# An attention and two-layer expert kernel: first weights of the second group's slots named by its first token, slots three steps earlier

## The chip, the cores and the metric

One core of a Trainium2 chip. The metric is the time of one execution in microseconds, lower is better; three runs of the kernel before are given, with their median.

## The reference

Three stages follow each other.

```python
# attention: q, k, v of 2 batches, 8 heads, 576 rows, 64 columns; top_k = 32
scores = scale * np.matmul(q, k.transpose(0, 1, 3, 2))
kth = np.partition(scores, -top_k, axis=-1)[..., -top_k:-top_k + 1]
scores = np.where(scores >= kth, scores, -1000000000.0)
attn = softmax(scores); x = attn @ v            # as x [1152, 512]
# first experts: one of 8 for each token
logits = x @ w_gate + modality_bias[modality_id]
e_idx = np.argmax(logits, axis=1)
out[mask] = gate_w[mask, None] * (np.maximum(x[mask] @ w1[e], 0.0) @ w2[e])
# second experts: all 4 for each token, weighted by domain_probs / sum
out += p[:, e:e + 1] * (np.maximum(x @ w1[e], 0.0) @ w2[e])
```

The hidden width is 1024, so one expert has w1 of 512x1024 and w2 of 1024x512, 2 MB each.

## The kernel before, in words

The 1152 tokens are nine tiles of 128. Attention runs over 72 "heads" g (nine query tiles of eight heads) in a loop of 78 steps p on each engine. In step p PE computes the scores of head p, multiplies head p-6 by the values and transposes head p-5. DVE finds the 32nd largest score of two heads at a time (find_thresholds, fourteen MAX8 and MATCH_REPLACE8 a pair), GpSimd masks (mask), ACT copies and takes exponents. Each engine has a generator beside(), advanced once a step (on DVE once behind each of the fourteen instructions, a clock of steps/7), which puts other work between the heads at written-out steps: A_START, TOKENS_AT and the like. Where no such work is due, PE multiplies v_one by itself (keep_dense, the filler).

The experts' tokens are sorted in two groups. Group A is tiles 0 to 2, and its first five slots (128 rows of one expert each, plain f32 matmuls) run inside the heads loop. A slot s takes seven steps from A_START + 7 s: a_x (transposes of gathered rows, a step ahead), up parts in three steps (3, 3 and 2 of eight), two a_turn (transposes), down parts in two steps (4 and 4); ACT copies between them (a_copy_xT, a_relu_half, a_copy_hT, a_copy_y). PE's clock inside the loop is held at step 75 and ACT's at 76, so that what is due later waits until the loop is over.

Group B is tiles 3 to 8. Its routing can only be finished with the last tile: pick finds each token's expert, ranks and more_ranks count tokens by matmuls with triangular matrices, place computes rows and slots of tokens, sum_tokens gives the list of tokens of each slot (tokens_made). Experts with tokens are served in the order of their numbers (kth_expert). Then GpSimd gathers the rows of the first two slots (gather_slot), PE transposes them (turn_slot), and each slot is computed with operands split in a rounded high part and a low part: ACT rounds (split_high, w1_high), DVE subtracts (split_low, w1_split), three matmuls for each product. Weights come through one raw buffer for w1 and one for w2, which group A's slots use too. SP issues the loads in program order: first_up for the first w1, held at its third quarter until tokens_made; w2 once the first rows have landed. Behind the slots come the four experts of the last stage for all tokens.

The seam from the last logits to slot 0 reads on PE:

```python
            last_logits()
            clock.now = AV_END - 1
            advance(work_beside)          # the fifth slot's last two up parts
            more_ranks(GB, GB.tiles - 1, 3)
            clock.now = AV_END + 2
            advance(work_beside)          # its two a_turn and four down parts
            sum_tokens(GB)
            clock.now = 1000
            for _ in work_beside:         # the other four down parts
                pass
```

## Time and profile before

| what | value |
|---|---|
| median of 3 runs | 943.93 us (943.23 to 944.47) |
| profiled execution, whole | 945.33 us |
| its span | 943.6 us |
| mean granted clock of PE | 0.962 |
| PE busy | 903.5 us, 96% of the span |
| DVE busy | 560.5 us, 59% |
| ACT busy | 340.5 us, 36% |
| GpSimd (POOL) busy | 280.8 us, 30% |

The rows are of the profiled execution, which took 945.33 us in all with a span of 943.6 from its first to its last instruction. Busy shares are means over stages: the heads loop ends near 416 us, group B's slots begin near 435 us and the last stage near 540 us. A granted clock of 1.00 is 2.4 GHz, one of 0.50 is 1.2 GHz. In the rows, an engine's time is followed by a line of the kernel, the operation, and output and inputs by name; a bracket gives the engine's idle time ahead of it and what ended that.

### The profile page before, as it was taken

The numbers are of one execution on the slowest core, as the hardware profiler recorded it, in microseconds if no ns is written. First come the engines' busy times: TensorE is split into PE (matmuls) and PEld (weight loads), VectorE is DVE, ScalarE is ACT, GpSimd is POOL, SyncE is SP. The second block draws the span as 40 slices with busy tenths as digits, with TensorE's granted clock in tenths as the row PEclk, the third lists the DMA queues.
The fourth block names the chain that finished last, engine by engine and source line by source line (L and its number), as shares of the span: only waits on it lengthen the run. The fifth ranks groups of instructions, "written<-read, shape, count | busy, mean of one in ns | idle before, by whom it ended". The sixth has DMA issues, their size and how long they took to land.

```text
span 943.6 us, 13457 instructions
## 1 busy us (share of the span) xinstructions
PE 903.5 (96%) x4823; PEld 758.8 (80%) x4823; DVE 560.5 (59%) x1097; ACT 340.5 (36%) x726; POOL 280.8 (30%) x227
## 2 busy tenths in 40 slices
PE   4999999998999999996999799999999999999998
PEld 4888888886676676764778689989998999889897
DVE  4999999999999998935544523324223421332121
ACT  3545555554454663524543412303112220222010
POOL 7576657655667666303111210000000000000000
PEclk8589999998899999997999899999999999999999
DMA  9130000005034353338916250022002200000001
GB/s 220 39 124 23 1 24 12 12 13 201 15 109 136 124 176 113 102 117 310 344 34 223 74 198 1 1 89 90 1 1 90 84 5 0 0 0 0 33 11 56
DMA packets 49396, 75.63 MB, mean 80 GB/s; under 512 B 24624, under 2 KB 24624, under 8 KB 49328
## 3 DMA queue, kind: packets, MB, share of 16 engines
q1 hardware_dynamic: 42160, 61.09, 19.1%
q0 software_dynamic: 4160, 13.63, 4.4%
q8 instruction: 36, 0.59, 0.3%
q10 hardware_dynamic: 3008, 0.05, 0.2%
q14 instruction: 32, 0.26, 0.1%
HBM read 63.49 MB, written 11.27 MB: 79 GB/s over the span
## 4 chain that ended last, share of the span: by engine, by line
PE 76%; DVE 17%; DMA 2%; issue 2%; POOL 1%; ACT 1%; SPq 0%; ACTq 0%; DVEq 0%; POOLq 0%
PE bank L1339 19%; PE bank L1341 18%; PE bank L1340 18%; DVE work L1038 7%; PE bank L1395 6%; DVE top L1043 5%; PE bank L1467 4%; PE bank L1334 3%; PE bank L1483 3%; PE bank L1366 2%; DVE top L1029 2%; PE bank L1364 1%; PE bank L1496 1%; DMA b_xs_raw<-x_dram,b_tok_i 1%; DMA w_raw<-in_moe_w_dram 1%
## 5 line engine op out<-in xcount | busy, mean ns | idle before, releaser
L620 POOL TENSOR_SCALAR att<-sc,top 128x576 f32<-128x576 f32 x70 | 120.6, 1723 | 122.5 <-DVE top L1043 119.8
L1043 DVE MAX8 top<-work 128x8 f32<-128x576 f32 x216 | 152.1, 743 | 0.1
L1339 PE MATMUL bank<-xT,w1h 128*128 128x384 f32 x384 | 129.6, 338 | 5.3 <-DVE w1l L1218 5.3
L1276 DVE SCALAR_TENSOR_TENSOR hT<-bank,hT 128x384 fp32r<-128x384 f32 x96 | 53.0, 557 | 131.0 <-ACT hT L940 129.0
L1341 PE MATMUL bank<-xT,w1h 128*128 128x384 f32 x384 | 129.1, 336 | 0.0
L1340 PE MATMUL bank<-xT,w1l 128*128 128x384 f32 x384 | 129.1, 336 | 0.0
L940 ACT ACTIVATE hT<-bank 128x384 fp32r<-128x384 f32 x96 | 46.9, 491 | 200.9 <-PE bank L1341 199.3
L1339 PE MATMUL bank<-w2h,hT 128*128 128x512 f32 x288 | 112.2, 390 | 1.2 <-DVE hT L1276 1.2
L1395 PE MATMUL bank<-v_one,attT 128*128 128x65 f32 (+3 forms) x800 | 111.8, 280 | 0.8 <-ACT av L752 0.6
L1341 PE MATMUL bank<-w2l,hT 128*128 128x512 f32 x288 | 112.2, 390 | 0.0
L1340 PE MATMUL bank<-w2h,hT 128*128 128x512 f32 x288 | 112.2, 389 | 0.0
L1395 PEld LDWEIGHTS bank<-v_one,attT 128*128 128x128 f32 (+3 forms) x800 | 97.7, 188 | 17.0 <-issue 9.3
L1038 DVE MATCH_REPLACE8 work<-top,work 128x576 f32<-128x576 f32 x144 | 106.3, 744 | 0.0
L623 POOL TENSOR_TENSOR att<-att,ex 128x576 f32<-128x576 f32 x70 | 98.8, 1412 | 7.2 <-ACT ex L738 1.6
L1288 DVE SCALAR_TENSOR_TENSOR x_tok<-bank,pr_e,x_tok 128x512 f32<-128x512 f32 x27 | 20.3, 751 | 115.0 <-PE bank L1341 115.0
L744 ACT ACTIVATE attT<-bank 128x512 f32<-128x512 f32 x72 | 43.0, 597 | 105.1 <-PE bank L1366 105.1
L1339 PEld LDWEIGHTS bank<-xT,w1h 128*128 128x128 f32 x384 | 72.8, 189 | 6.0 <-DVE w1l L1218 5.7
L1340 PEld LDWEIGHTS bank<-xT,w1l 128*128 128x128 f32 x384 | 72.8, 189 | 0.3
L1341 PEld LDWEIGHTS bank<-xT,w1h 128*128 128x128 f32 x384 | 72.6, 189 | 0.0
L729 ACT ACTIVATE sc<-bank 128x576 f32<-128x576 f32 x72 | 46.6, 647 | 68.4 <-PE bank L1341 68.4
L1339 PEld LDWEIGHTS bank<-w2h,hT 128*128 128x128 f32 x288 | 54.1, 188 | 12.5 <-DVE hT L1276 1.5
L1341 PEld LDWEIGHTS bank<-w2l,hT 128*128 128x128 f32 x288 | 54.0, 188 | 11.3
(253 smaller groups left out, 1520.4 us busy)
## 6 DMA issues: line engine op xcount, KB each, us to landing
w_raw<-in_moe_w_dram SPq DMA_DIRECT2D x96, 512.0 KB, 6.3
q_raw<-in_q_dram SPq DMA_DIRECT2D x18, 128.0 KB, 2.6
v_one<-in_v_dram POOLq DMA_DIRECT2D x18, 128.0 KB, 5.6
out_dram<-x_tok SPq DMA_DIRECT2D x9, 256.0 KB, 2.0
k_raw<-in_k_dram SPq DMA_DIRECT2D x8, 256.0 KB, 5.2
y_dram<-zero POOLq DMA_DIRECT2D x2, 1024.0 KB, 6.7
y_dram<-b_ys POOLq DMA_DIRECT2D x7, 256.0 KB, 3.4
x_dram<-x_cur SPq DMA_DIRECT2D x6, 256.0 KB, 2.1
```

The lines of the kernel that those rows point to most:

```text
L620: nc.gpsimd.tensor_scalar(att[:, g % ATR, :], sc[:, g % RING, :], top8[:, g % RING, 3, 7:8], None, ALU.is_ge).then_inc(keep_made, 1)
L623: nc.gpsimd.tensor_tensor(att[:, g % ATR, :], att[:, g % ATR, :], ex[:, g % EXR, :], ALU.mult).then_inc(att_made, 1)
L729: nc.scalar.activation(sc[:, g % RING, :].rearrange("p (a b) -> p a b", a=2), bank[:, SB:SB + 2, 0:HS], ACT.Copy, scale=float(D) ** -0.5). ...
L744: nc.scalar.activation(attT[:, g % 2, 0:KC - 1, :].rearrange("p c q -> p (c q)"), bank[:, TBK, :], ACT.Copy)
L940: nc.scalar.activation(hTh(b)[:, f, :], bank[:, HB + f % 4, 0:BW], ACT.Relu).then_inc(h_high, 1)
L1038: nc.vector.match_replace(out=work[:, j, :], in_to_replace=top8[:, g % RING, i, :], in_values=sc[:, g % RING, :] if i == 0 else work[:, j, ...
L1043: nxt = nc.vector.max(out=top8[:, g % RING, i + 1, :], in_=work[:, j, :])
L1276: nc.vector.scalar_tensor_tensor(out=hTl(b)[:, f, :], in0=bank[:, HB + f % 4, 0:BW], scalar=0.0, in1=f32(hTh(b)[:, f, :]), op0=ALU.max, op ...
L1339: nc.tensor.matmul(dst, high_lhs, high_rhs, start=start, stop=False)
L1340: nc.tensor.matmul(dst, low_lhs, high_rhs, start=False, stop=False)
L1341: return nc.tensor.matmul(dst, high_lhs, low_rhs, start=False, stop=stop)
L1395: last = nc.tensor.matmul(bank[r0:r1, AVB, 0:W], attT[0:kk, g % 2, c, r0:r1], v_one[b][0:kk, h, c, :], start=(c == 0), stop=(c == KC - 1))
```

## The change

Five things are changed together.

1. Group B's experts are numbered from the expert of its first token on (turn_experts): DVE takes that token's expert out of the first four tiles' pick, PE spreads it over all partitions by a matmul with a one-row matrix (spread_first, in step 72), and DVE makes from it first_i and the turned numbers that one-hots are compared with. place turns kth_expert back, now behind the slot tables.
2. SP's first_up waits for first_made instead of the second group's experts_made, and has no pause at the third quarter. The store of the last x tile moves behind it. ke is read behind the waits ahead of the first w2 load.
3. A_START goes from 46 to 43, TOKENS_AT from 42 to 40, place on DVE starts 0.6 step earlier and its second part is asked for at TOKENS_AT - 1.8; x transposes and logits of tiles 3 to 6 come two steps later.
4. On PE more_ranks of the last tile follows last_logits directly. With the slots three steps earlier, the fifth slot's up parts and a_turn are now inside the heads loop, and its down parts are what stands around sum_tokens.
5. GpSimd makes the low part of the first two w1 quarters; DVE makes that of the other two. ACT rounds all four at once, ahead of the first rows' copy and behind the beside work, and takes the second group's Exp behind that work too. The rare slots beyond the fifth move out of the generators.

```diff
@@ -208,9 +213,9 @@
         RING, EXR, ATR = 8, 4, 3
-        EXP_LAG, TR_LAG, AV_LAG, X_LAG, L_LAG = 2, 5, 6, 17, 18
+        EXP_LAG, TR_LAG, AV_LAG = 2, 5, 6
         STEPS = HEADS + AV_LAG
-        RANKS_AT, TOKENS_AT, A_START, A_STEP, SPREAD = 37, 42, 46, 7, 5
+        RANKS_AT, TOKENS_AT, A_START, A_STEP, SPREAD = 37, 40, 43, 7, 5
         HB, HTB, YB, XB = 0, 2, 4, 7
...
@@ -218,11 +223,15 @@
 
-        def x_at(p, lag):
-
-            t = (p - lag) // H
-            return t if p >= lag and (p - lag) % H == 0 and t < T - 1 else None
-
+        def x_at(p):
+
+            return next((t for t in range(T - 1) if p == t * H + (19 if TB <= t < T - 2 else 17)), None)
+
+        def logits_at(p):
+            return x_at(p - 1)
+
+        FIRST_AT = HEADS
+        AV_END = HEADS + AV_LAG - 1
         turn_use = {}
...
@@ -236,14 +245,14 @@
                 next_use("ql", low)
-            if x_at(p, X_LAG) is not None:
-                next_use("x", x_at(p, X_LAG))
-            if x_at(p, L_LAG) is not None:
-                next_use("lg", x_at(p, L_LAG))
+            if x_at(p) is not None:
+                next_use("x", x_at(p))
+            if logits_at(p) is not None:
+                next_use("lg", logits_at(p))
+            if p == FIRST_AT:
+                next_use("first", 0)
         next_use("x", T - 1)
         next_use("lg", T - 1)
-
-        AV_END = HEADS + AV_LAG - 1
 
...
@@ -466,13 +477,11 @@
 
-            def load(e, kth, raw, src, split, loaded, pause=False):
+            def load(e, kth, raw, src, split, loaded):
                 sp.wait_ge(split, kth * DC + BASE)
...
                 for c in range(DC):
-                    if pause and c == 2:
-                        sp.wait_ge(GB.tokens_made, 2)
                     sp.dma_start(raw[:, c * n:(c + 1) * n, :], rows[:, c * n:(c + 1) * n, :]).then_inc(loaded[c], 16)
...
@@ -483,8 +492,8 @@
             def first_up():
-                sp.wait_ge(GB.experts_made, 2)
-                load(expert_of(0), 0, w1_raw, w1, w1_split, w1_loaded, True)
+                sp.wait_ge(first_made, 1)
+                load(sp.value_load(first_i[0:1, 0:1], min_val=0, max_val=E - 1), 0, w1_raw, w1, w1_split, w1_loaded)
 
...
@@ -501,6 +510,7 @@
                 with sp.If(guarded(sp, GA, SPREAD)):
+                    keep_x(T - 1)
                     a_store(SPREAD - 1)
...
@@ -518,6 +528,7 @@
                     first_up()
+                    keep_x(T - 1)
                     a_store(SPREAD - 1)
...
@@ -536,21 +547,20 @@
                 clock.now = p
-                if x_at(p, X_LAG) is not None:
-                    keep_x(x_at(p, X_LAG))
+                if x_at(p) is not None:
+                    keep_x(x_at(p))
                 low = q_at(p)[1]
...
                 advance(work_beside)
-            keep_x(T - 1)
             clock.now = 1000
...
 
+            sp.wait_ge(a_d, GA.slots)
+            sp.wait_ge(slot_loaded[0], 16)
             ke = sp.value_load(GB.table_i[0:1, 1, E:E + 1], min_val=1, max_val=E)
-            sp.wait_ge(slot_loaded[0], 16)
-            sp.wait_ge(a_d, GA.slots)
             load(expert_of(0), 0, w2_raw, w2, w2_split, w2_loaded)
...
@@ -637,11 +650,6 @@
                 yield from clock.until(1000)
-                with pool.If(guarded(pool, GA, SPREAD)):
-                    for s in range(SPREAD, GA.slots):
-                        with pool.If(guarded(pool, GA, s)):
-                            a_gather(s)
-                            pool.sem_inc(passed, 1)
                 pool.wait_ge(a_stored, 16 * GA.slots)
...
@@ -657,6 +665,14 @@
                 advance(work_beside)
+            with pool.If(guarded(pool, GA, SPREAD)):
+                for s in range(SPREAD, GA.slots):
+                    with pool.If(guarded(pool, GA, s)):
+                        a_gather(s)
+                        pool.sem_inc(passed, 1)
+            for c in range(2):
+                pool.wait_ge(w1_high, c + 1)
+                nc.gpsimd.tensor_tensor(w1l[:, c, :], w1_raw[:, c, :], f32(w1h[:, c, :]), ALU.subtract).then_inc(w1_split, 1)
             pool.wait_ge(x_kept, 16 * T)
...
@@ -815,24 +831,22 @@
                 a_copy_y(SPREAD - 1)
-                yield from clock.until(1000)
-                with act.If(guarded(act, GA, SPREAD)):
-                    for s in range(SPREAD, GA.slots):
-                        with act.If(guarded(act, GA, s)):
-                            a_copy_xT(s)
-                            a_relu_half(s, 0)
-                            a_relu_half(s, 1)
-                            a_copy_hT(s, 0)
-                            a_copy_hT(s, 1)
-                            a_copy_y(s)
-                            act.sem_inc(passed, 1)
-                        with act.Else():
-                            act.drain().then_inc(a_xT_copied, 1)
-                            act.drain().then_inc(a_relu, 2)
-                            act.drain().then_inc(a_hT_copied, 2)
-                            act.drain().then_inc(a_ys, 1)
-                with act.Else():
-                    act.drain().then_inc(a_ys, GA.slots - SPREAD)
+
+            def a_rare_slots():
+                for s in range(SPREAD, GA.slots):
+                    with act.If(guarded(act, GA, s)):
+                        a_copy_xT(s)
+                        a_relu_half(s, 0)
+                        a_relu_half(s, 1)
+                        a_copy_hT(s, 0)
+                        a_copy_hT(s, 1)
+                        a_copy_y(s)
+                        act.sem_inc(passed, 1)
+                    with act.Else():
+                        act.drain().then_inc(a_xT_copied, 1)
+                        act.drain().then_inc(a_relu, 2)
+                        act.drain().then_inc(a_hT_copied, 2)
+                        act.drain().then_inc(a_ys, 1)
 
...
@@ -870,19 +884,24 @@
                     act.wait_ge(zero_set, 1)
-            read_rest_of_x()
-            act.wait_ge(GB.lsub_made, 3)
-            nc.scalar.activation(GB.lg_b[:, :, :], GB.lg_a[:, :, :], ACT.Exp).then_inc(GB.lexp_made, 1)
-            clock.now = 1000
-            for _ in work_beside:
-                pass
-
             def split_high(kth, raw, high, loaded, done, parts=range(DC)):
...
                     nc.scalar.activation(high[:, c * n:(c + 1) * n, :], raw[:, c * n:(c + 1) * n, :], ACT.Copy).then_inc(done, 1)
+
+            read_rest_of_x()
+            clock.now = 1000
+            for _ in work_beside:
+                pass
+            act.wait_ge(GB.lsub_made, 3)
+            nc.scalar.activation(GB.lg_b[:, :, :], GB.lg_a[:, :, :], ACT.Exp).then_inc(GB.lexp_made, 1)
+            with act.If(guarded(act, GA, SPREAD)):
+                a_rare_slots()
+            with act.Else():
+                act.drain().then_inc(a_ys, GA.slots - SPREAD)
+            split_high(0, w1_raw, w1h, w1_loaded, w1_high)
 
...
@@ -919,12 +938,10 @@
 
-            split_high(0, w1_raw, w1h, w1_loaded, w1_high, (0, 1))
             act.wait_ge(GB.table_made, 2)
...
             slot_xT(0)
-            split_high(0, w1_raw, w1h, w1_loaded, w1_high, (2, 3))
             split_high(0, w2_raw, w2h, w2_loaded, w2_high)
...
@@ -1099,8 +1116,23 @@
                     dve.wait_ge(g.rank_made, 1)
-                nc.vector.tensor_tensor(g.onehot[:, a:b, :], over_e(g.lidx[:, a:b], n), over_t(ecol_less[:, :], n), ALU.is_equal).then_inc(g.hot_made, 1)
+                if g is GB and part == 1:
+                    yield from turn_experts(step)
+                names = turned_less if g is GB else ecol_less
+                nc.vector.tensor_tensor(g.onehot[:, a:b, :], over_e(g.lidx[:, a:b], n), over_t(names[:, :], n), ALU.is_equal).then_inc(g.hot_made, 1)
                 yield
+
+            def turn_experts(step):
+
+                nc.vector.tensor_copy(first_less[:, :], GB.lidx[:, 0:1]).then_inc(first_seen, 1)
+                yield from clock.until(HEADS - 1.6)
+                dve.wait_ge(turn_made, turn_use["first", 0])
+                nc.vector.tensor_copy(first_less[:, :], bank[:, TXB, 0:1]).then_inc(turn_read, 1)
+                dve.wait_ge(turn_read, turn_use["first", 0])
+                nc.vector.tensor_scalar(first_i[:, :], first_less[:, :], float(E), None, ALU.add).then_inc(first_made, 1)
+                step(nc.vector.tensor_scalar(turned_less[:, :], ecol[:, :], first_less[:, :], None, ALU.add))
+                step(nc.vector.tensor_scalar(turned_by[:, :], turned_less[:, :], 0.0, -float(E), ALU.is_ge, ALU.mult))
+                step(nc.vector.tensor_tensor(turned_less[:, :], turned_less[:, :], turned_by[:, :], ALU.add))
 
...
@@ -1111,7 +1143,7 @@
                 step(nc.vector.tensor_reduce(out=g.lidx[:, t:t + 1], in_=g.lg_a2[:, t, :], axis=AX.X, op=ALU.min))
-                nc.vector.tensor_scalar(g.onehot[:, t, :], ecol_less[:, :], g.lidx[:, t:t + 1], None, ALU.is_equal).then_inc(g.hot_made, 1)
+                nc.vector.tensor_scalar(g.onehot[:, t, :], turned_less[:, :], g.lidx[:, t:t + 1], None, ALU.is_equal).then_inc(g.hot_made, 1)
                 nc.vector.tensor_scalar(g.lg_a[:, t, :], lp, g.lmax[:, t:t + 1], None, ALU.subtract).then_inc(g.lsub_made, 1)
...
@@ -1133,7 +1165,8 @@
                 step(nc.vector.tensor_reduce(out=g.kth_expert[:, :], in_=g.cmp_kth[:, :, :], axis=AX.X, op=ALU.add))
-                nc.vector.tensor_copy(g.kth_expert_i[:, :], g.kth_expert[:, :]).then_inc(g.experts_made, 1)
+                if g is GA:
+                    nc.vector.tensor_copy(g.kth_expert_i[:, :], g.kth_expert[:, :]).then_inc(g.experts_made, 1)
                 yield
...
@@ -1161,6 +1194,10 @@
                 nc.vector.tensor_copy(g.by_slot_i[:, 1, :], g.by_slot[:, 1, :]).then_inc(g.table_made, 1)
+                if g is GB:
+                    step(nc.vector.tensor_scalar(g.kth_expert[:, :], g.kth_expert[:, :], first_less[:, :], None, ALU.add))
+                    step(nc.vector.tensor_scalar(turned_by[:, :], g.kth_expert[:, :], 0.0, float(E), ALU.is_lt, ALU.mult))
+                    nc.vector.tensor_tensor(g.kth_expert_i[:, :], g.kth_expert[:, :], turned_by[:, :], ALU.add).then_inc(g.experts_made, 1)
                 yield from tokens_asked
...
@@ -1175,8 +1212,8 @@
                 yield from pick(GA, 0, TB, 1)
-                yield from clock.until(RANKS_AT - 0.4)
-                yield from place(GA, 1, clock.until(TOKENS_AT - 2.2))
+                yield from clock.until(RANKS_AT - 1)
+                yield from place(GA, 1, clock.until(TOKENS_AT - 1.8))
                 yield from clock.until(HEADS - 4)
...
@@ -1261,9 +1298,9 @@
             ke = dve.value_load(GB.table_i[0:1, 1, E:E + 1], min_val=1, max_val=E)
-            split_low(0, w1_raw, w1h, w1l, w1_high, w1_split, (0, 1))
+            dve.wait_ge(w1_split, 2 + BASE)
+            split_low(0, w1_raw, w1h, w1l, w1_high, w1_split, (2, 3))
             slot_xT_low(0)
-            split_low(0, w1_raw, w1h, w1l, w1_high, w1_split, (2, 3))
             split_low(0, w2_raw, w2h, w2l, w2_high, w2_split)
...
@@ -1406,6 +1443,13 @@
                 last.then_inc(turn_made, 1)
+
+            def spread_first():
+
+                pe.wait_ge(first_seen, 1)
+                pe.wait_ge(zero_set, 3)
+                take_turn("first", 0)
+                nc.tensor.matmul(bank[:, TXB, 0:1], first_row[:, :], first_less[:, :], start=True, stop=True).then_inc(turn_made, 1)
 
...
@@ -1628,17 +1672,17 @@
                     transpose_att(p - TR_LAG)
-                if x_at(p, L_LAG) is not None:
-                    x_logits(x_at(p, L_LAG))
+                if logits_at(p) is not None:
+                    x_logits(logits_at(p))
                 advance(work_beside)
+                if p == FIRST_AT:
+                    spread_first()
                 if p == HEADS + 2:
...
             last_logits()
+            more_ranks(GB, GB.tiles - 1, 3)
             clock.now = AV_END - 1
-            advance(work_beside)
-            more_ranks(GB, GB.tiles - 1, 3)
-            clock.now = AV_END + 2
             advance(work_beside)
...
```

## Rows read from the trace of the kernel before

**Rows 1.** Busy time by stretch: PE, PEld, DVE, ACT, POOL, PEclk, DMA share, GB/s

```profile
245.00:264.50 19.50, 19.50 (x84) 13.12 (x82) 19.50 (x42) 9.29 (x25) 13.51 (x10) 0.82 0.09 29
...
245.30:416.30 171.00, 169.88 (x920) 120.11 (x918) 151.68 (x325) 87.77 (x223) 96.24 (x64) 0.98 0.36 120
...
429.20:434.70 5.50, 0.00 (x0) 0.00 (x0) 2.36 (x2) 2.60 (x3) 0.09 (x1) 0.85 0.83 229
434.70:443.40 8.70, 7.15 (x19) 5.49 (x20) 6.02 (x6) 5.66 (x6) 4.53 (x4) 0.51 0.84 293
...
448.20:453.70 5.50, 5.50 (x24) 4.57 (x25) 4.81 (x6) 4.62 (x6) 0.23 (x1) 1.00 1.03 406
```

**Rows 2.** Chain of waits over the seam: start us, us, what

```profile
416.31 3.40 PE bank L1467 x4
...
420.09 0.21 DVE b_cmp_cnt L1124
...
423.78 0.96 DVE b_row_hot L1153
...
427.00 7.62 DMA b_xs_raw<-x_dram,b_tok_i
...
444.50 1.06 ACT w2h L885
```

**Rows 3.** Timelines of DVE, ACT and PE in the seam: start us, us, engine

```profile
417.01 0.23 DVE L1114 TENSOR_SCALAR b_onehot<-ecol_less,b_lidx 128x8 f32<-128x8 f32 x1
...
431.71 2.36 DVE L1218 TENSOR_TENSOR w1l<-w_raw,w1h 128x1024 fp32r<-128x1024 f32 x2 [4.93 <-ACT w1h L885]
...
417.40 0.24 ACT L875 ACTIVATE b_lg_b<-b_lg_a 128x48 f32<-128x48 f32 x1 [1.64 <-DVE b_lg_a L1115]
...
429.20 0.60 ACT L792 ACTIVATE ys<-bank 128x512 f32<-128x512 f32 x1 [7.52 <-PE bank L1483]
430.62 2.00 ACT L885 ACTIVATE w1h<-w_raw 128x1024 fp32r<-128x1024 f32 x2 [0.82 <-issue]
...
425.49 3.68 PE L1483 MATMUL bank<-w_raw,hsT 128*128 128x512 f32 x8
```

**Rows 4.** Groups of instructions on GpSimd: busy us, mean ns | idle us

```profile
L623 POOL TENSOR_TENSOR att<-att,ex 128x576 f32<-128x576 f32 x70 | 98.8, 1412 | 7.2 <-ACT ex L738 1.6
...
L577 POOL TENSOR_TENSOR q_raw<-q_raw,q_high 128x512 f32<-128x512 f32 x9 | 11.5, 1279 | 4.3 <-ACT q_high L706 4.3
```

**Rows 5.** Timelines of PE and GpSimd around steps 41 to 45

```profile
218.99 1.11 PE L1334 MATMUL bank<-ident,x_cur 128*128 128x128 f32 x4 [4.59 <-DVE x_cur L1067]
...
229.90 0.40 PE L1339 MATMUL bank<-kTh,qTh 64*128 64x288 f32 x1
...
233.19 1.04 PE L1496 MATMUL bank<-v_one 128*128 128x260 f32 x4
...
244.25 0.30 PE L1364 MATMUL bank<-ident,att 128*64 128x128 f32 x1 [1.87 <-POOL att L623]
...
222.64 1.41 POOL L623 TENSOR_TENSOR att<-att,ex 128x576 f32<-128x576 f32 x1
```

**Rows 6.** Gathers to landing: all of xs_raw, b_xs_raw at 427.0, at 473.7

```profile
DMA to landing us min/median/max: 3.4/6.3/7.1
...
b_xs_raw<-x_dram,b_tok_i POOLq DMA_INDIRECT x1, 7.6
...
b_xs_raw<-x_dram,b_tok_i POOLq DMA_INDIRECT x1, 3.4
```

**Rows 7.** Timelines of PE and DVE near the loop's end

```profile
392.03 0.60 PE L1334 MATMUL bank<-ident,x_cur 128*128 128x128 f32 x4
...
400.08 0.96 PE L1407 MATMUL bank<-wg,gxT 128*128 128x8 f32 x8
...
406.41 0.30 PE L1364 MATMUL bank<-ident,att 128*64 128x128 f32 x1
...
387.47 1.41 DVE L1029 MAX8 top<-sc 128x8 f32<-128x576 f32 x2
```

26 lines of the change are left out of this document (18 added, 8 removed).

## The prediction

> **What bounds the kernel now.** I read the busy time by stretch first [rows 1]. Between 245.3 and 416.3 us, the last 32 steps of the heads loop with the first group's slots woven in, PE is busy 169.88 of 171.00 us: it is the bound, so PE work moved inside this stretch keeps its price. Behind it comes the seam to the second group's slots: 429.2 to 434.7 has no PE work at all, and 434.7 to 443.4 has a granted clock of 0.51, the 1.2 GHz level of the two (1.2 and 2.4).
>
> Then the chain of waits over the seam [rows 2]. The last logits end at 416.3; slot matmuls of 3.40 us stand ahead of the ranks; DVE places the tokens from 420.09 on, with the rows' one-hot done at 424.74; GpSimd issues the first row gather at 427.00, and it is the transfer, 7.62 us, that PE waits for. The timelines of the engines [rows 3] show what stands beside: the last matmul of the first group ends at 429.17 (425.49 + 3.68), ACT copies ys until 429.80, and only at 430.62 rounds the first w1 quarter; DVE subtracts from 431.71. Today none of this is last, as w1 is ready before the gathered rows are.
>
> **Part 1: two w1 quarters go to GpSimd, ahead of the gather.** This is the part that decides. In GpSimd's program the new loop waits for the first and second w1_high and subtracts each quarter; only behind it stand the waits for the tokens and gather_slot(0). On ACT, w1_high still comes behind all of the beside work, whose last piece, a_copy_y of the fifth slot, waits for a_d, the end of that slot's eight down parts. PE issues the second four of them behind sum_tokens, as before. So w1, fetched early, isn't rounded early. The chain to the gather becomes: down parts, ys, the second group's Exp (now behind ys), w1h, two subtractions on GpSimd, gather.
>
> Its length [rows 3]: ys ends 0.63 after the down parts; 0.82 of issue as today; Exp 0.24; w1h until who waits for it can start 1.09 (430.62 to 431.71). The subtraction of 128x1024 on GpSimd is not in the trace. The nearest rows are the same operation on 128x512 (1279 ns) and 128x576 (1412 ns) [rows 4]: 2.08 ns an element, so 1024 take 1.28 + 512 x 0.00208 = 2.35 us; by doubling it would be 2.56. The low end is DVE's 1.2 for this shape (two in 2.36 [rows 3]), which GpSimd reaches in no row. I take 2.35, twice, 4.7; the second w1h is hidden under the first subtraction. With 0.3 to issue: 0.63 + 0.82 + 0.24 + 1.09 + 4.7 + 0.3 = 7.8 us from the end of the down parts to the gather. There is a rule on this choice of engine: the Trainium skill, "GPSIMD Engine Reference", Engine selection, gives two-input elementwise work to VectorE, GpSimd being about twice as slow. By it a subtraction is 2 x 1.2 = 2.4 us and the chain 0.1 longer; it speaks against this part, and the two rows bear it out.
>
> **Part 2: slots three steps earlier, ranks ahead of the last portion.** How does the end of the down parts move? I keep a ledger of PE from the start of step 43, now 229.90 [rows 5].
> - The first slot's transposes now stand in step 42 and wait for its rows. GpSimd can issue that gather behind mask 37, whose product ends at 224.05 (222.64 + 1.41), so at 224.4. The 4 MB of weights, issued some 5 us earlier than now, are still in flight. This gather took 6.3 as a median, bounds 3.4 and 7.1 [rows 6]. Rows at 230.7, transposes 0.6: step 43 starts at 231.3, +1.4.
> - Dense filler of steps 43 and 44 goes, 1.0 each: -2.0. The idle 1.87 at 244.25 is filled: -1.9. The 0.6 of transposes is now ahead of step 43: -0.6.
> - x transposes and logits of tile 3, two steps later than now, fall into 43 and 44: 0.5 + 0.8 [rows 7] = +1.3.
> - Two up parts and eight transposes now stand ahead of the last logits. By the rate of the down parts (3.68 for eight) four such matmuls are 1.8 at full clock (3.4 today in the seam, where the clock drops), the transposes 0.9: +2.7.
> - spread_first, one small matmul: 0.3; in step 76 nothing but the last heads covers ACT's copy of attT: some 0.4: +0.7.
>
> Sum +1.6: the last logits end near 418.0. The low clock behind 244.25 (0.82 over 19.5 us [rows 1], so 7.0 us at half speed, 3.5 lost) I leave in, since PE idles ahead of step 43 instead. Behind the logits PE waits 0.93 for DVE's last one-hot (416.31 to 417.24 today), the ranks and the hand-over take 0.6: DVE starts to place at 419.5, against 420.09. Then 4.7 to sum_tokens as now, 0.7 for it, 3.7 for the last down parts: they end at 428.6 against 429.2. What three steps of lead gain is nearly all paid back, as PE is the bound on both sides: -0.6.
>
> DVE's new work: turn_experts has six instructions like the 0.23 of 417.01, 1.2 us with their waits, and the second of them waits for PE's step 72. PE reaches its end some 6 us after DVE's place, since it has steps 71 and 72 with three up parts each in between. DVE idles so long; behind it are eleven passes of 0.70 (the rest of the pair and the first product), 7.7 + 1.2 = 8.9 us. PE has from step 73 to head 70's transposes 392.03 to 406.41 now, 14.4 [rows 7], of which 7.0 is slot work (3.7 + 2.8 + 0.5) that shrinks to 2.4: 9.8. So the wait is covered, by 0.9. The three instructions put ahead of tokens_made (0.5 us) leave it near 427, 9 us ahead of the gather; nobody waits.
>
> **Part 3: the gather and slot 0.** The gather starts at 428.6 + 7.8 = 436.4, 9.4 later than now. But the w1 load is over by then, and w2 is held until these rows land: the gather runs with no weights beside it. Today's took 7.6 us with w1 quarters in flight; a later one with the queues empty took 3.4 [rows 6]. A second gather follows 1.3 us behind, so I take 3.6, bounds 3.4 and 7.6: rows at 440.0 against 434.6, +5.4. What follows is as now, the low clock after an idle stretch too. w2's first issue has one register load more ahead of it (0.3) and less traffic beside it; the chain goes through w2's rounding (444.50) with the up parts ending beside it, so half a microsecond either way: nothing.
>
> **Part 4: the new numbering.** The slots of an expert are filled by its own tokens, so their number and that of weight sets stay. Changes of expert fall ahead of other slots, perhaps twice in succession. Ahead of slot 1 that is so today, a slot after the first load, and PE is busy 5.50 of 5.50 us up to it [rows 1]. Nothing.
>
> **Sum.** -0.6 for the down parts, +10.0 for the gather (427.0 was 2.2 ahead of their end and is now 7.8 behind), -4.0 for its transfer: +5.4 us. The rows are of an execution with a span of 943.6 that took 945.33 in all; the median of three is 943.93, and I add to that: **949.3 us**.
>
> **Rivals.**
> - *PE's slack is worth all it shows* (the other side). Idle 4.59 and 1.87, four fillers of 1.04 and 3.5 of low clock between 212 and 264 [rows 1, 5], 14 us, would leave the path and the down parts end that much earlier: 943.9 + 6.0 - 14 = 936. It decides from about 8 us. Against it: PE's idle at 218.99 is a wait for DVE's x_cur, and heads 36 to 39 are held by DVE whatever PE does. 0.06.
> - *Half of it is*: the first slot's gather lands soon enough, step 43 starts as now and PE doesn't cool, 1.4 + 3.5 less: 944.4, no change to be measured. 0.12.
> - *The gather stays slow*: four more gathers are issued within 6 us behind it. At 7.6 us: 953.3. 0.14. The Trainium skill, "DMA: Bandwidth & Descriptors", Latency and other measured facts, has HBM latency at 2 us under load and 0.2 without: by that the gather would gain 1.8 and the time be 951.5. The row of 3.4 says more.
> - *DVE's new wait comes on the path*: its cover is 0.9 of a sum of a dozen terms. Without it most of the 6 us shows in the last logits, about 954. 0.10.
> - The forecast has 0.58. That the change doesn't do what it says is part of it: nobody waited for w1, so its early fetch alone is worth nothing.
>
> **How the numbers follow.** A measurement of this kernel tells 0.2%, 1.9 us, from no change: 942.0 to 945.8. From the cases: faster 0.06, within 0.12, slower 0.82. The range goes from 945, into the half case, to 955, past the slow gather and DVE's wait; some 0.12 is left below and 0.05 above. The forecast's own range, from the subtraction's 2.56 and a step or two of PE, is 947 to 952.
>
> **What would show it.** GpSimd: two subtractions of about 2.35 us ending just ahead of the first b_xs_raw gather, near 436, which lands in under 4 us. ACT: w1h behind ys, though w1 landed before 415. PE: idle some 11 us ahead of slot 0. DVE: a wait of several us in the last pair of heads. I am wrong if the down parts end before 422, if w1h comes ahead of them, or if the gather takes 7 us.

## The result, and the profile after

The changed kernel takes 956.09 us as a median (953.17 to 961.23, four executions) against 943.73 us for the kernel before in the same measurement: ratio 1.0136, 95% interval 1.0091 to 1.0181. It is slower, by 12.4 us, where the forecast had 5.4 and the range ended at 955. The profiled execution has a span of 951.4 us against 943.6, so 7.8 of the 12.4 are in this trace; the rest lies between executions.

Busy time of the changed kernel by stretch (PE, PEld, DVE, ACT, POOL, granted clock, DMA share, GB/s); the fourth row answers to the idle stretch in [rows 1], the fifth to the one behind it:

```profile
229.90:245.30 15.40, 15.40 (x90) 10.98 (x89) 15.40 (x35) 7.47 (x18) 12.97 (x9) 0.82 0.06 18
245.30:416.10 170.80, 169.33 (x957) 120.47 (x955) 148.67 (x323) 90.14 (x227) 93.52 (x62) 1.00 0.38 132
416.10:428.20 12.10, 11.12 (x27) 5.42 (x26) 7.00 (x34) 0.00 (x0) 0.00 (x0) 0.72 0.04 15
428.20:440.10 11.90, 0.12 (x1) 0.00 (x0) 2.93 (x5) 4.62 (x6) 8.42 (x5) 0.72 0.18 51
440.10:453.70 13.60, 8.81 (x28) 6.63 (x28) 4.80 (x5) 5.30 (x7) 2.99 (x4) 0.75 0.94 335
```

PE has nothing to do for 11.9 us where it had nothing for 5.5. The timelines of ACT, POOL, PE and SP in the seam, to be laid beside [rows 3]:

```profile
417.98 6.24 PE L1527 MATMUL bank<-w_raw,hsT 128*128 128x512 f32 x8
...
428.36 0.60 ACT L808 ACTIVATE ys<-bank 128x512 f32<-128x512 f32 x1 [12.68 <-PEq L1591]
428.85 0.23 ACT L899 ACTIVATE b_lg_b<-b_lg_a 128x48 f32<-128x48 f32 x1
429.77 3.90 ACT L892 ACTIVATE w1h<-w_raw 128x1024 fp32r<-128x1024 f32 x4 [0.69 <-issue]
430.91 4.64 POOL L675 TENSOR_TENSOR w1l<-w_raw,w1h 128x1024 fp32r<-128x1024 f32 x2 [37.00 <-ACT w1h L892]
435.59 2.36 DVE L1255 TENSOR_TENSOR w1l<-w_raw,w1h 128x1024 fp32r<-128x1024 f32 x2 [5.83 <-POOL w1l L675]
435.71 2.02 POOL L680 DMA_INDIRECT b_xs_raw<-x_dram,b_tok_i  x1 [0.16 <-issue]
...
440.23 1.09 PE L1371 MATMUL bank<-ident,b_xs_raw 128*128 128x128 f32 x4 [11.91 <-DMA b_xs_raw<-x_dram,b_tok_i]
441.46 14.99 SPq L485 DMA_DIRECT2D w_raw<-in_moe_w_dram  x12
```

ACT waits 12.68 us for the last down part while w1, whose four loads were all issued by 404.4 and landed within 6.3 us, lies ready; the rounding follows, then the two subtractions (2.32 us each), and only then the gather. PE waits 11.91 us for it. The chain of waits shows the two transfers and what stands between them, beside [rows 2]:

```profile
435.71 4.38 DMA b_xs_raw<-x_dram,b_tok_i
...
440.17 0.27 SPq L563
...
443.18 8.98 DMA w_raw<-in_moe_w_dram
...
452.18 1.06 ACT w2h L892
453.24 0.49 ACT b_hs L927
```

The rows land 5.5 us later than before (440.09 against 434.62), but w2's last quarter is rounded 7.7 us later (452.18 against 444.50 [rows 2]), and the relus come behind it. Beside w2's fetch stand the first group's token gathers (x_tok). In the kernel before, the first of them came 1.39 us behind w2's first issue at 435.34; in the changed kernel, whose first issue is at 441.46, it comes 2.17 us ahead of it. The fetch and the first gather of the kernel before, then the gathers of the changed kernel:

```profile
437.05 7.43 DMA w_raw<-in_moe_w_dram
...
436.73 0.95 POOL L647 DMA_INDIRECT x_tok<-y_a,a_pos_i  x1 [7.44 <-DMA y_a<-ys]
```

```profile
439.29 0.95 POOL L655 DMA_INDIRECT x_tok<-y_a,a_pos_i  x1 [0.31 <-issue]
440.55 0.95 POOL L655 DMA_INDIRECT x_tok<-y_a,a_pos_i  x1 [0.30 <-issue]
441.80 0.95 POOL L655 DMA_INDIRECT x_tok<-y_a,a_pos_i  x1 [0.30 <-issue]
```

### The profile page after: what moved, and what is told of

Read it like the earlier page. It is cut to its first block, busy times and chain, and to the rows that moved or that the text cites. A ratio compares the mean times of both kernels' runs of the same rounds, so it can differ in the third digit from the quotient of the medians.

```text
span 951.4 us, 13448 instructions
## 1 busy us (share of the span) xinstructions
PE 903.7 (95%) x4813; PEld 758.7 (80%) x4813; DVE 557.8 (59%) x1103; ACT 340.6 (36%) x726; POOL 286.1 (30%) x231
## 4 chain that ended last, share of the span: by engine, by line
PE 75%; issue 10%; POOL 9%; DMA 3%; SPq 1%; DVE 1%; ACT 1%; PEld 1%; PEldq 0%; POOLq 0%; DVEq 0%; ACTq 0%
PE bank L1376 19%; PE bank L1377 18%; PE bank L1378 18%; PE bank L1432 6%; POOL att L633 6%; PE bank L1511 4%; PE bank L1371 4%; PE bank L1527 3%; POOL att L636 2%; PE bank L1403 2%; PE bank L1401 1%; DMA w_raw<-in_moe_w_dram 1%; DMA q_raw<-in_q_dram 1%; DMA xs_raw<-x_a,a_tok_i 1%; PE bank L1540 1%
```

## The experiments

All times are medians of all executions; each ratio is against the kernel before on the same chip, with a 95% interval. It can differ by up to 0.2% from the quotient of the two medians. "Profile" is one execution of each. The runs are on three chips, so a step between two kernels of different chips is better read from the ratios.

**The changed kernel again**, to have it on one chip with the next two and the first of those that hold w1 back:

> The changed kernel, unchanged. Its profile showed a span of 951.4 us, but its other executions took 955 to 961. If the spread lies in the seam (where the w2 load, the gathers and the next w1 load meet), this profile shows the last w2 quarter landing at another distance from its issue than 10.7 us, and the rest of the kernel, from slot 0's first down product on, at 494.8 us as before. If it lies in the last stage instead, that stretch differs. Median expected: 956, lowest to highest 6 us or more apart, while the kernel before stays within 1.5.

955.78 us, ratio 1.0103 (1.0077 to 1.0130), the kernel before 944.64. The profiled execution is a middle one, span 954.8: 3.4 us more than the profile shown above. 2.0 are there at 308.9 us already (the transposes of one of the first group's row blocks start at 308.88 instead of 306.92), 1.6 at slot 0's first down product (457.86 instead of 456.27), and 1.8 come behind that, where the granted clock from 455 to 500 us is 0.93 instead of 0.97. The seam isn't where the two differ, and the kernel before doesn't stay within 1.5 us as expected: its 23 executions are 7.3 us apart (941.8 to 949.1).

**GpSimd's subtractions behind the first two gathers:**

```
-for c in range(2): (wait for w1_high; w1l[:, c] = ...)   # GpSimd
 gather_slot(0)
 gather_slot(1)
+for c in range(2): (wait for w1_high; w1l[:, c] = ...)
```

> The changed kernel with GpSimd's two subtractions moved behind the first two gathers. Queue theory (the gather waits for work put ahead of it on GpSimd): gather at 425.8 instead of 435.7, rows at about 430; then slot 0 waits for the rest of the w1 split on DVE (end 438) and starts near 438.7 against 442.8; w2 issued 10 us earlier lands by 441 and no longer delays the down parts, which start near 449.5 against 456.6: 7 us off the changed kernel, about 949. Rival, that the loss lies in the heads loop (DVE's wait for step 72, slots moved): the time stays at 956 and only idle time shifts.

947.38 us, ratio 1.0031 (1.0008 to 1.0053): 8.4 us less than the changed kernel, 6.8 by the two ratios. The gather and the turn of its rows:

```profile
427.74 1.05 POOL L677 DMA_INDIRECT b_xs_raw<-x_dram,b_tok_i  x1 [32.02 <-DVE b_pos_i L1204]
...
431.30 0.63 PE L1371 MATMUL bank<-ident,b_xs_raw 128*128 128x128 f32 x4 [1.73 <-DMA b_xs_raw<-x_dram,b_tok_i]
```

Part 1 has its price shown: what stands ahead of the gather on GpSimd is most of the loss.

**ScalarE rounds the first w1 as soon as the last x is read**, subtractions left ahead of the gather:

```
 read_rest_of_x()
+split_high(0, w1_raw, w1h, w1_loaded, w1_high)
 (the rest of the first group)
```

> The changed kernel with ACT's rounding of the first w1 moved ahead of the last beside work (the copy of ys), all else the same. Queue theory: w1h at 415.8 to 419.7, subtractions on GpSimd end near 421.5, before the tokens are known at 425; the gather goes at 425.8, rows near 430, slot 0 at 432.8 against 442.8, down parts near 444 to 445 against 456.6: 12 us off, about 943 or somewhat below the kernel before (938 to 943). Heads-loop rival: no better than 950.

946.72 us, ratio 1.0021 (1.0003 to 1.0039), where 938 to 943 was expected. That is 9.1 us less than the changed kernel: rounding early takes off the same wait as moving the subtractions, so the two gains are one and don't add. The gather comes at 429.29, 3.5 us later than expected. 1.4 of that are there before the tokens are placed (the one-hot step starts at 418.25 here, at 416.82 in the changed kernel's profile). For the other 2 the timelines say why, first of this kernel:

```profile
417.93 4.66 POOL L675 TENSOR_TENSOR w1l<-w_raw,w1h 128x1024 fp32r<-128x1024 f32 x2 [22.94 <-ACT w1h L892]
...
418.25 2.06 DVE L1146 TENSOR_SCALAR b_onehot<-turned_less,b_lidx 128x8 f32<-128x8 f32 x1
...
421.98 0.78 DVE L1160 TENSOR_TENSOR b_cmp_pre<-below,b_counts 128x144 f32<-128x144 f32 x1
```

and the same two VectorE steps in the kernel with the gather first, where GpSimd is idle beside them:

```profile
419.00 0.23 DVE L1146 TENSOR_SCALAR b_onehot<-turned_less,b_lidx 128x8 f32<-128x8 f32 x1
...
420.90 0.31 DVE L1160 TENSOR_TENSOR b_cmp_pre<-below,b_counts 128x144 f32<-128x144 f32 x1
```

Beside GpSimd's subtractions a step of 0.23 us took 2.06, and it ends with the first of them; another took 0.78 instead of 0.31 and ends with the second. The six other VectorE steps beside them kept their lengths. All of them belong to the steps that make the token lists. VectorE's own two quarters then stood behind the Exp and were made at 434.75.

**All four low quarters on VectorE again:**

```
-for c in range(2): ...                          # GpSimd
-dve.wait_ge(w1_split, 2 + BASE)
-split_low(0, w1_raw, ..., (2, 3))
+split_low(0, w1_raw, ...)
```

> Undoes one part of the change alone: VectorE makes all four low quarters of the first w1, as before, and GpSimd makes none, so that the gather of slot 0 stands behind nothing but its tokens. Against the kernel with the two gathers ahead of GpSimd's subtractions (947.4 us): there VectorE waited for GpSimd until 436.9, made its two quarters by 439.2 and only then the low part of the rows (439.8). Theory (the seam is bound by what stands in one engine's line): the four quarters of 1.2 us each follow ScalarE's (431.0 to 434.9) and end at about 436.2, the low part of the rows at 437.0, first product 437.2 instead of 440.0, first down product about 2.5 us earlier; time about 945. Rival (GpSimd's help is worth its time, since VectorE has four subtractions of w2 to make as well): 947 to 948. A second rival (the second product waits for w2 and not for the rows): first product 3 us earlier but down product at the same place, time 947.

946.87 us, ratio 1.0032 (1.0018 to 1.0045). The first product starts at 437.98, 0.8 later than by the theory, the second at 447.11, 1.1 us before that of the kernel before; yet the median is 3 us above it. (The profiled execution took 945.65 us.) So the seam of one profile doesn't give the median any more, and the help of GpSimd is worth nothing measurable: 1.0032 against 1.0031.

**The first group's steps as before**, alone in the changed kernel:

```
-RANKS_AT, TOKENS_AT, A_START = 37, 40, 43    (x of tiles 3 to 6 at step 19)
+RANKS_AT, TOKENS_AT, A_START = 37, 42, 46    (x at step 17, and the other engines' steps)
```

> The changed kernel with the first group's steps as in the kernel before (ranks 37, tokens 42, first slot from 46, x of each tile at its step 17, and the steps of GpSimd, ScalarE and VectorE with them); all else as changed. Against the changed kernel on this chip (955.8). Theory A (the moved steps bring TensorE to the lower clock: 0.50 in 222 to 230 us and 0.70 to 0.82 in 230 to 245, where before it was 0.82 and 1.00): the loop over the heads ends 1 to 3 us earlier, time 953 to 955. Theory B (my ledger: the moved steps take 1.5 to 2 us of waits out of TensorE's line before the end of the down parts): time 957 to 958. Nothing in the seam itself changes by either.

960.25 us, ratio 1.0184 (1.0159 to 1.0209): 4 to 5 more than either measurement of the changed kernel. That is theory B's direction, 2 us above its range. In its profile eight transposes and sixteen down products are left behind the token sums, and ys comes at 432.97 instead of 428.36.

**These steps alone in the kernel before:**

> The kernel before, with only the first group's steps and the step of each x as in the changed kernel (tokens 40, first slot from 43, x of the tiles from the fourth to the seventh two steps later, ranks asked 0.6 of a step earlier); no new numbers, no early fetch of w1, no ranks ahead, GpSimd makes no low quarters. In the changed kernel these steps are worth 4.3 us (960.3 without them). Theory A (they take waits out of TensorE's line wherever they stand): down parts end 2 to 3 us earlier; the gather waits for the tokens at the same place as before, which come 1 to 2 us earlier too: time 941 to 943. Theory B (they pay only with the ranks ahead, since their other price is the lower clock of 222 to 245 us): 944 to 946.

949.90 us, ratio 1.0060 (1.0037 to 1.0082). Neither theory: it costs 5.8 us. Its timelines:

```profile
416.56 5.38 PE L1485 MATMUL bank<-w_raw,hsT 128*128 128x512 f32 x8
...
421.78 0.28 PE L1444 MATMUL bank<-b_onehot,before 128*128 128x8 f32 x2
...
425.86 0.60 ACT L794 ACTIVATE ys<-bank 128x512 f32<-128x512 f32 x1 [7.82 <-PE bank L1485]
...
429.23 1.05 POOL L666 DMA_INDIRECT b_xs_raw<-x_dram,b_tok_i  x1 [33.98 <-DVE b_pos_i L1169]
```

The down parts end 3.3 us earlier, as the theory has it, but eight of their products now stand ahead of the last ranks, where four up products stood [rows 2], so the ranks come 2.2 us later, and with them tokens and gather (429.23 against 427.00). Slot 0's first down product is 3.6 us later (451.74 against 448.18), 1.9 of it in w2's fetch, which took 9.28 us here instead of 7.43. The moved steps pay only with the ranks ahead. What the ranks ahead do by themselves isn't shown: no run has them alone.

**The next w1 held back until the first w2 is rounded; the three x_tok gathers behind slot 1; both together:**

```
+sp.wait_ge(w2_high, DC)                      # SyncE, ahead of the other experts' loads
 gather_slot(1)
-(gathers of x_tok)
+(slot(0), slot(1)), then (gathers of x_tok)  # GpSimd
```

> The changed kernel with SP holding the second expert's w1 load until the first w2 is rounded. Load theory (w2's 10.7 us to landing come from the next w1 load beside it): last w2 quarter lands 7 to 9 us after the first issue, slot 0's down parts start 2 to 3 us earlier, median 953. Rival, that the three x_tok gathers and the third row gather beside it make w2 late: 10 to 11 us as before, median unchanged at 956.

> The changed kernel with the three gathers of the first group's rows (x_tok) put behind GpSimd's work of slot 1, so that they no longer run beside the load of the first w2. Theory (the fetch of w2 took 10.7 us from first issue to last quarter because these gathers share the DMA engines with it, 200 to 250 GB/s where 400 were reached later): w2 lands within about 8.5 us of its first issue, the second product begins 1.5 to 2 us earlier, time about 954. Rival (the fetch is slow for itself, or the low clock of TensorE holds the product as long): w2's time stays 10 us or the down product stays where it was, time 956.

> The changed kernel with both loads kept from the fetch of the first w2: the gathers of the first group's rows behind slot 1, and the second expert's weights behind the rounding of w2. Each alone left the fetch at 9.0 and 10.4 us from first issue to last landing (10.7 in the changed kernel). If the two share it: about 7.5 us, its 2 MB at some 400 GB/s and 2 us until the first bytes; the second product is then bound by the first one and begins at about 451. If the fetch is slow for itself: 9 us again. The time itself gains at most 1 to 2 us by it, since slot 1 waits for the gathers of the tokens: 953 to 956.

957.79, 955.91 and 959.73 us, ratios 1.0129 (1.0104 to 1.0153), 1.0135 (1.0105 to 1.0164), 1.0148 (1.0123 to 1.0172): none gains. The chain of waits gives the time from w2's last issue to its landing, of the three in turn:

```profile
450.06 8.68 DMA w_raw<-in_moe_w_dram
```

```profile
442.02 7.25 DMA w_raw<-in_moe_w_dram
```

```profile
449.23 6.87 DMA w_raw<-in_moe_w_dram
```

It was 8.98 in the changed kernel, and 7.43 in the kernel before (its last issue at 437.05, landed at 444.48). Four profiles with the changed kernel's order from there on (this one, its second, that with the old steps, that with products at steps 74 and 75) have 8.98, 9.20, 8.74 and 8.83. So the gathers of the tokens cost the fetch some 1.7 us, and the 0.3 to 0.4 of the next w1 are no more than two executions differ. In the second kernel the down products start 3.3 us earlier (452.96 against 456.27), 1.1 of which are there at its gather already, and the end gets nothing: from there to the end it takes 498.6 us instead of 495.1, 1.9 of them a wait of slot 1 for its relu. That is the expectation's own remark on the third kernel, true of the second too.

**All low quarters on VectorE, old steps, late token gathers:**

> The three edits together: all four low quarters on VectorE, the first group's steps as before, the first group's rows gathered behind slot 1. What then is left of the change: the new numbers of the experts, the early fetch of w1, and the ranks ahead of the slot portions. If the parts add up: 945 less 1 to 3 of the steps (theory A) less about 0.5 of the gathers (w2 is not the last there) gives 942 to 944, at or a little under the kernel before (944.6). If the steps cost nothing (theory B): 946 to 947.

952.60 us, ratio 1.0082 (1.0059 to 1.0105). Neither of the expected ranges has it. 5.7 more than with the low quarters alone: the old steps' price once more.

**Early rounding without GpSimd's part, then early register reads, then products to fill PE's wait:**

```
 read_rest_of_x()
+act.wait_ge(GB.lsub_made, 3); Exp
+split_high(0, w1_raw, w1h, w1_loaded, w1_high)
 (the first group's last copies)
...
+sp.wait_ge(GB.experts_made, 2)
+ke = sp.value_load(...); first = expert_of(0)
 sp.wait_ge(a_d, GA.slots)
 sp.wait_ge(slot_loaded[0], 16)
...
+12 x matmul(bank[:, MB, 0:P], ident, ident)
 turn_slot(0)
+12 x matmul(bank[:, MB, 0:P], ident, ident)
```

> The kernel with all low quarters on VectorE (946.9 us), and ScalarE's Exp and its rounding of the first w1 put ahead of the fifth slot's last copies, as soon as the last x is read. It tells what ScalarE's order costs once GpSimd stands in nobody's way. Theory (the seam is bound by what stands in ScalarE's line, and GpSimd's half caused the poor gain of the kernel that rounded early, where a VectorE step took 2.06 us instead of 0.23 beside GpSimd's subtraction): rounding from about 418 to 422, VectorE's four quarters done by 431, low part of the rows at 432 instead of 437.2, first product 432.5 instead of 438.0; then w2 (first issue 432, last quarter 440.5) is what the second product waits for: it begins at 442 to 443 instead of 447.1. Time 942 to 943. Rival (the second product and all after it hang on w2's fetch, which does not move): first product 5 us earlier, time 945 to 947.

> The kernel before this one, and SyncE reads the number of experts and the first expert into its registers before it waits for the last down part and the gather (the changed kernel reads them behind both waits: 1.3 to 1.7 us from the landing to the first issue). If the second product waits for w2: w2's first issue 1.0 to 1.3 us earlier and the time 1 us less than the kernel before this one. If the rows or TensorE's clock are what it waits for: no difference.

> The kernel before this one, and TensorE makes 12 products of the unit matrix with itself before it turns the first rows and 12 behind (0.13 us each at the full clock, into a bank that nobody reads), so that it does not stand still between the last down part and the first product. If the low clock in the seam costs (0.50 while the first product runs, 4.3 us for what takes 2.7 at the full clock): the first product runs at the full clock and ends 2 to 3 us earlier; if the second one then waits for w2 all the same, the time is only 0 to 1 us less. If the clock falls nevertheless: 0 to 1 us more, for the products before the rows' turn.

945.80, 944.38 and 946.54 us; ratios 1.0019 (1.0001 to 1.0037), 0.9999 (0.9981 to 1.0016), 1.0030 (1.0009 to 1.0052). The second is the best version found; it is level with the kernel before, not ahead of it. In the first one's profile the first product starts at 433.02 (expected 432.5), 5 us earlier than with the low quarters alone, and the second at 444.79 (expected 442 to 443), only 2.3 earlier; the median gains about 1 us. In the second kernel's profile the first product starts at 432.90, 4.4 us before that of the kernel before, and the gain ends there:

```profile
442.46 1.06 ACT L891 ACTIVATE w2h<-w_raw 128x1024 fp32r<-128x1024 f32 x1 [2.10 <-DMA w_raw<-in_moe_w_dram]
443.43 1.07 ACT L926 ACTIVATE b_hs<-bank 128x512 f32<-128x512 f32 x2
```

The relus stand behind w2's last quarter on ACT. Its first issue is 431.34, as without the early reads (431.39), but ys starts 0.46 us later in this profile: from ys to the issue it is 2.85 us instead of 3.36, half a microsecond of the 1.0 to 1.3 expected. From the last issue to the landing it took 9.38 us instead of 7.99. How long it takes goes with how closely the token gathers follow w2's first issue: where the first of them comes 0.3 to 0.8 us behind it, the fetch took 9.3 to 9.8 us (this kernel, that with the fillers, the steps alone in the kernel before); where it comes 1.05 to 4 us behind, 6.2 to 8.1 (six kernels, the kernel before among them; one profile each). Two of those six, with 6.2 and 6.7 us, also issue the next w1 late, behind a wait of 2 to 3 us, and no run moves the distance alone, so this is a pattern and not a shown cause. With the fillers the first product runs at the full clock and takes 5.7 us (436.81 to 442.5) instead of 7.4, but it starts 3.9 us later, 2.3 of which are there at ys and the rest is its wait for the fillers: they buy nothing. Each filler is two instructions and took 0.24 us (12 in 2.94), not 0.13.

**The relus ahead of w2's last two quarters; the same with the next w1 held:**

```
-split_high(0, w2_raw, w2h, ...)              # four quarters, ahead of slot 0
+split_high(0, w2_raw, w2h, ..., (0, 1)); slot 0: relu, relu, split_high(..., (2, 3)), ...
```

> The kernel with early rounding, VectorE's low quarters and the early register reads (944.4 us), and in ScalarE's line the last two quarters of the first w2 stand behind the two relus of slot 0 instead of ahead of them. In the trace of that kernel the relus start one quarter behind the last quarter of w2 (443.4 us), while the first half of the product they read was ready at about 437 and the second at 440.3. Theory (the fetch of w2 holds the second product through ScalarE's order, not through the weights that its first parts need): relus at 437.5 and 441, first down product at about 443 instead of 446.6; the product then waits a little for the last quarters; time 941.5 to 942.5. Rival (the last quarters of w2 are needed at the same time anyway, since the product lasts only 5.5 us at the full clock): down product begins 3 us earlier and stands still in its middle; time 943.5 to 944.5.

> The kernel before this one, and SyncE's loads of the second expert's weights wait until ScalarE has rounded all of the first w2. If the next w1 slows the last quarters of w2 (here the gathers of the rows and tokens come early, at 426 to 436, so that they do not hide it): w2's last quarter lands about 2 us sooner and the time is 1 to 2 us less than the kernel before this one. If it does not (as in the changed kernel with the same wait): same time within 1 us.

947.41 and 946.91 us, ratios 1.0033 (1.0016 to 1.0051), 1.0031 (1.0015 to 1.0047). In the second's profile the first relu is at 439.61, but the two quarters now stand ahead of the copies of the turned h on ACT, and the down product starts at 447.01, no sooner than the 446.58 of the kernel without. The wait only moved one instruction on. PE stands 3.28 us ahead of the down product, which then takes 8.4 us (to 455.45), the first half at the low clock, instead of 5.9 (to 452.43). By the ratios both kernels are some 3 us slower than the one without, outside both of the expected ranges.

**The clock.** Ten products between the last logits and the ranks:

> The kernel with the relus sooner, and ten products of the unit matrix with itself (0.13 us each at the full clock) between the last logits and the ranks. There TensorE stands for 1.0 us in all kernels with the ranks ahead, and the first four of the fifth slot's down parts then run at the low clock: eight instructions in 5.4 to 6.7 us, where the kernel before took 3.67. If the standing still is what brings the low clock: these eight take 3.7 to 4 us, the down parts end at 427 instead of 428.3 (the slot portions, on VectorE, then set the second half's start), time 1 us less than the kernel without. If not: the same clock, and up to 0.5 us more.

949.80 us, ratio 1.0052 (1.0033 to 1.0071), 2.4 more than without them. The eight products of the down parts behind them take 3.68 us instead of 6.07; but the ten fillers take 4.12 us themselves, at the low clock, and cost more than they give:

```profile
423.07 6.07 PE L1527 MATMUL bank<-w_raw,hsT 128*128 128x512 f32 x8
```

```profile
421.84 4.12 PE L1685 MATMUL bank<-ident 128*128 128x128 f32 x20
...
426.17 3.68 PE L1527 MATMUL bank<-w_raw,hsT 128*128 128x512 f32 x8
```

That the stand of 1 us ahead of them brings the low clock isn't shown: with the steps alone in the kernel before, the down parts follow the last logits without it and the first eight take 5.38 us, and in the kernel before it is the four up parts there that take 3.54 us, where four take 1.88 at the full clock. Whatever large products come first behind the last heads' small ones ran in part at the low clock in these profiles. Its profile showed something else: the clock had fallen long before. The stretch 408 to 416 us of this kernel, of the kernel with the relus sooner, of that with w2 alone, and of the changed kernel above:

```profile
408.00:416.00 8.00, 7.81 (x36) 7.02 (x36) 1.89 (x10) 2.42 (x8) 0.00 (x0) 0.51 0.30 119
```

```profile
408.00:416.00 8.00, 7.81 (x36) 7.17 (x36) 1.25 (x5) 2.72 (x9) 0.00 (x0) 0.50 0.22 88
```

```profile
408.00:416.00 8.00, 7.81 (x38) 7.01 (x37) 2.32 (x10) 1.99 (x6) 0.00 (x0) 0.54 0.34 137
```

```profile
408.00:416.00 8.00, 6.87 (x53) 5.91 (x51) 1.72 (x8) 3.57 (x11) 0.00 (x0) 1.00 0.23 93
```

In four of the fourteen profiles with the moved steps and the ranks ahead (the fourth is that with the next w1 held) the granted clock goes to 0.50 between 407 and 411, before the last logits, and ys comes at 433 to 436 instead of 427 to 432. The code up to there is the same in all of them. So two more runs put six products of 128 x 260 into steps 74 and 75:

```
 if p == HEADS + 2: ranks(GB)
+if p in (HEADS + 2, HEADS + 3):
+    pe.wait_ge(a_ys, SPREAD - 1)
+    keep_dense(MB + 2, 3)
```

> The changed kernel with six products of 128 x 260 more on TensorE (three at step 74, three at 75), where the kernel before had six up parts of the fifth slot and the changed one has only small products from 401.8 us on. In the four profiled executions that are 4 to 6 us longer up to the last logits (last logits at 419.7 to 421.4 instead of 415 to 416.8) the granted clock falls to 0.50 at 407 to 411, in the others at 415 to 418. Theory (the moved steps took the large products away from here, and the clock then falls in some executions before the last logits): no execution has the early fall, none is over 957, the median is 952 to 954 in spite of 1.2 us of work more. Rival (the fall has another reason, and products that do nothing are only work more): the early fall still comes in some, median 957.

> The same six products in the kernel with early rounding, VectorE's low quarters and the early register reads (944.4 us, 940.8 to 949.3 in 12 executions). Theory: its executions of 945 to 949 are those with the early fall of the clock; they vanish, its spread is 3 us, the median 942 to 943.5, under the kernel before. Rival: 945.5, spread as it was.

956.83 us (956.04 to 958.50 in four executions), ratio 1.0133 (1.0108 to 1.0157), and 945.34 us (941.33 to 949.65 in twelve), ratio 1.0012 (0.9992 to 1.0031). Both profiles have the full clock up to 416, but two of the first kernel's four executions are over 957, the second kernel's lie as far apart as without the fillers (8.3 us against 8.4), and neither median falls. The early fall is real where it shows; it isn't shown to be what spreads the times. The theory fails in its main point.

## Why the prediction was wrong, step by step

- **Part 1, the gather behind the subtractions: right.** From the end of the down parts (428.32) to the gather at 435.71 it is 7.39 us, predicted 7.8. A subtraction took 2.32, predicted 2.35 from [rows 4]; VectorE's took 1.18 for the same shape. By the Trainium skill, "GPSIMD Engine Reference", Engine selection, GpSimd is about twice as slow, and the trace agrees (1.97 times). Taking them from ahead of the gather gave 8.4 us back by the medians, 6.8 by the ratios.
- **Part 2, the end of the down parts: right by two misses.** It was 428.3, predicted 428.6. The last logits end at 416.1 and VectorE starts to place at 418.16, predicted 418.0 and 419.5: the ledger was 1.3 to 1.9 too long. But the first eight down products took 6.24 us instead of 3.67, at the low clock. In the kernel before that price fell on the four up parts in this place (3.54 us); the sum took them at 1.8 once they were moved away, and didn't see that the low clock stays and meets what stands there now. VectorE waits 5.90 us for PE's step 72, predicted 6, and head 70's transposes start at 407.62 behind ranks that left no gap: covered.
- **Part 3, the rows: right.** Landed at 440.09, predicted 440.0; the transfer took 4.38 us with no weights in flight, predicted 3.6, against 7.62 beside weights. The 0.8 goes with the issuing instruction: behind the subtractions it takes 2.02 us on GpSimd, where it took 1.05 in the kernel that rounds early without GpSimd's part, and the transfer there took 3.52. The other price, an estimate of 1.8 us of gain from the Trainium skill's "DMA: Bandwidth & Descriptors", Latency and other measured facts (HBM latency of 2 us at high load, 0.2 on average), was too little: it gained 3.2.
- **Part 3, "w2's first issue ... and less traffic beside it; half a microsecond either way: nothing": the step that failed.** It cost 2.6 us in the trace: slot 0's first down product starts 8.1 us later (456.27 against 448.18), with the rows 5.5 later. From the rows' landing to the last issue of w2 it was 3.09 us instead of 2.43, since the register loads now stand behind the wait. From there to the landing it was 8.98 instead of 7.43: there isn't less traffic beside w2 but more, because the gather came so late that the first group's token gathers, once 1.4 us behind w2's first issue, were issued ahead of it and beside it. With these gathers moved away it took 7.25. And the transposes of h ran at the low clock (from the last rounding's end to the first down product 3.0 us instead of 2.6), as PE stood still between the first product and the late relus. The prediction had put the chain through w2's rounding, and didn't ask what its new neighbours were.
- **Part 4: right.** Slots follow each other by 13.1 us in both kernels, and from the first down product to the end it is 495.1 against 495.4.
- **The sum.** Forecast +5.4 on the path; the trace has 5.5 for the rows, 2.6 for w2 and -0.3 behind: +7.8. The other 4.5 are between executions: the profiled one of the kernel before took 945.33, 1.6 us more than this measurement's median of 943.73, which the prediction had said (as 1.4) before it set the difference on the median; that of the changed kernel took 953.17, 2.9 less than its median. The sum had no term for this, and it is the larger part of the miss of 6.8. Either term alone would have left the time inside the range that ended at 955: 949.3 with 2.6 more is 951.9, with 4.5 more 953.8, both estimates. And I took TensorE's clock to stay as it was ("The low clock behind 244.25 I leave in"). Behind PE's wait at 219 us it is 0.50 in 222 to 230 us in the changed kernel where it was 0.82, and behind that it differs between executions of the same code. The stretch from 230 us in the profile shown, and then in the second profile of the same kernel, which is 2.0 us later at 308.9:

```profile
230.00:245.00 15.00, 15.00 (x89) 10.81 (x89) 15.00 (x31) 7.47 (x18) 12.57 (x9) 0.82 0.06 19
```

```profile
230.00:245.00 15.00, 15.00 (x82) 10.63 (x80) 15.00 (x32) 5.68 (x13) 12.55 (x9) 0.69 0.07 19
```

- **The rivals.** "PE's slack is worth all" and "half of it" didn't happen. "The gather stays slow" and "DVE's wait on the path" didn't either. The nearest times, 953.3 and about 954, were given for reasons that aren't the case.

Of the 11.1 us on one chip (955.8 against 944.6), GpSimd's place costs 8.4 (6.8 by the ratios), and it costs this only together with the late rounding: with either undone the wait is gone. 2 to 3 us are left. They go as ScalarE rounds early and SyncE reads early (946.9, 945.8, 944.4; ratios 1.0032, 1.0019, 0.9999), but the steps of 1.1 and 1.4 are about the size of their intervals, so neither share is shown. What remains of the change, taken together (new numbers, early fetch, ranks ahead, moved steps), gives and costs nothing that these runs can tell: 0.9999 (0.9981 to 1.0016).

Left open: why executions of one kernel lie 6 to 8 us apart (942.7 to 948.5 in sixteen of the kernel before, 953.2 to 961.2 in four of the changed one), and so which of them a single profile shows. TensorE's clock differs between executions in two places of the trace; keeping it up in the later one didn't narrow the times of the twelve executions (four of the changed kernel are too few to tell), and the earlier one (222 to 245 us) wasn't tried by itself.

## What to carry to other kernels

Fetching something early is worth nothing while the instruction that uses it stands behind a later wait on its own engine: follow the datum through every engine's order down to the last user. Nothing that waits belongs ahead of a gather on GpSimd's queue. When a step on the chain is shifted by several microseconds, list anew which transfers now fall beside the next one, and don't take over its duration; and where large products follow a stretch of small ones and short waits, count the first of them at the clock that the trace shows in that place, whatever stood there before. Widen the range by what two executions of the same code differ.
